# Delta rule and two FFNs on one core: when the second FFN's weights are prepared

## What is computed

```python
# 1: delta rule, B 4, H 8, S 768, D 48
k_n = k / (norm(k) + 1e-6)
for t in range(S):
    y[:, :, t] = einsum('bhd,bhde->bhe', q[:, :, t], state)
    v_old = einsum('bhde,bhd->bhe', state, k_n[:, :, t])
    state = state + beta[t] * einsum('bhd,bhe->bhde', k_n[:, :, t], v[:, :, t] - v_old)
x = y as (3072 tokens, 384)
# 2: first FFN, d_ff 2048
h = maximum(x @ w_in, 0.0);  x = (h * h) @ w_out
# 3: second FFN, d_ff 1536
out = (1 / (1 + exp(-(x @ w_gate))) * (x @ w_val)) @ w_last
```

## Time and profile before

| | us |
|---|---|
| median of 3 runs (lowest, highest) | 992.91 (991.66, 994.58) |
| the profiled execution's own time | 993.12 |
| its span | 991.3 |
| PE busy | 946.8 (96%) |
| DVE busy | 655.4 (66%) |
| ACT busy | 515.1 (52%) |
| POOL busy | 12.4 (1%) |
| mean granted clock of PE, of full speed | 0.987 |

### The profile page before, as it was taken

One profiled execution on the slowest core, in us unless ns is written; L12 is line 12 of the kernel. 1 busy time (PEld: TensorE's weight loads), 2 busy tenths in 40 slices (PEclk: granted clock), 3 DMA queues, 4 the chain that ended last, 5 costly groups with the idle time before them and its releaser, 6 DMA issues.

```text
span 991.3 us, 24647 instructions
## 1 busy us (share of the span) xinstructions
PE 946.8 (96%) x10372; PEld 518.8 (52%) x10372; DVE 655.4 (66%) x1260; ACT 515.1 (52%) x903; POOL 12.4 (1%) x27
## 2 busy tenths in 40 slices
PE   2878999999999999999999999999999999999998
PEld 1464555565565456556544445555555555555554
DVE  7998966965866885694236744675565655756745
ACT  4896655766576476556669843233333333232332
POOL 0000000000000000000000000000000000000000
PEclk7899999999999999999999999999999999999999
DMA  9633016024003202201133010010010010100000
GB/s 311 127 81 84 2 35 129 34 67 96 34 19 81 67 33 66 65 33 41 59 121 135 1 64 1 1 63 0 0 63 0 0 63 0 35 28 0 32 1 33
DMA packets 21001, 52.23 MB, mean 53 GB/s; under 512 B 2672, under 2 KB 12912, under 8 KB 20528
## 3 DMA queue, kind: packets, MB, share of 16 engines
q1 hardware_dynamic: 20320, 50.60, 18.0%
q10 hardware_dynamic: 592, 0.33, 0.1%
HBM read 41.48 MB, written 9.44 MB: 51 GB/s over the span
## 4 chain that ended last, share of the span: by engine, by line
PE 83%; DVE 9%; ACT 3%; issue 3%; DMA 1%; SPq 0%; POOL 0%; DVEq 0%; POOLq 0%; ACTq 0%
PE psum L699 72%; PE psum L613 2%; DMA raw_a<-in_w_in 1%; ACT work L833 1%; PE psum L600 1%; DVE attn L1212 1%; PE psum L570 1%; DVE attn L1210 1%; PE psum L557 1%; PE psum L582 1%; PE psum L628 1%; PE psum L544 1%; PE psum L642 1%; PE psum L509 1%; DVE work L1256 1%
## 5 line engine op out<-in xcount | busy, mean ns | idle before, releaser
L699 PE MATMUL psum<-work,w 128*128 128x512 f16 x1728 | 387.9, 381 | 9.6 <-DVE work L1256 4.1
L699 PE MATMUL psum<-attn 128*128 128x512 f16 x1296 | 285.4, 379 | 0.0
L699 PEld LDWEIGHTS psum<-work,w 128*128 128x128 f16 x1728 | 164.7, 98 | 206.3 <-issue 8.2
L833 ACT ACTIVATE work<-work 128x512 f16<-128x512 f32 (+1 forms) x264 | 155.8, 624 | 154.4 <-DVE work L1459 150.8
L699 PEld LDWEIGHTS psum<-attn 128*128 128x128 f16 x1296 | 126.8, 98 | 145.7 <-DVE attn L1285 1.3
L1459 DVE SCALAR_TENSOR_TENSOR work<-psum,work 128x512 f32<-128x512 f32 x72 | 49.8, 691 | 134.5 <-PE psum L699 120.2
L833 ACT ACTIVATE work<-psum,scal 128x512 f32<-128x512 f32 x90 | 60.1, 682 | 81.4 <-PE psum L699 81.4
L1256 DVE SCALAR_TENSOR_TENSOR work<-work 128x512 f16<-128x512 f16 x96 | 65.7, 689 | 52.1 <-ACT work L833 50.7
L833 ACT ACTIVATE attn<-psum 64x384 f32<-64x384 f32 (+5 forms) x160 | 65.8, 441 | 50.6 <-PE psum L570 21.0
L833 ACT ACTIVATE work<-psum 128x512 f32<-128x512 f32 x96 | 57.0, 594 | 66.7 <-PE psum L699 65.6
L699 PE MATMUL psum<-work,attn 128*128 128x256 f16 (+1 forms) x540 | 87.9, 315 | 0.0
(11 more groups left out here) (119 smaller groups left out, 747.3 us busy)
## 6 DMA issues: line engine op xcount, KB each, us to landing
attn<-in_kt SPq DMA_DIRECT2D x24, 192.0 KB, 4.0
attn<-in_v SPq DMA_DIRECT2D x24, 192.0 KB, 3.9
attn<-in_kn SPq DMA_DIRECT2D x24, 192.0 KB, 3.9
x_spill<-work SPq DMA_DIRECT2D x6, 768.0 KB, 3.3
xt<-x_spill SPq DMA_DIRECT2D x6, 768.0 KB, 5.0
attn<-in_qt SPq DMA_DIRECT2D x20, 192.0 KB, 4.3
y_out<-work SPq DMA_DIRECT2D x5, 768.0 KB, 3.6
work<-in_w_out SPq DMA_DIRECT2D x1, 3072.0 KB, 24.1
```

What stands on the lines that cost most here:

```text
L699: m = mm(dst, x, z, start=first and i == 0, stop=last and i == len(a) - 1)
L833: return nc.scalar.activation(out, in_, f, scale=scale)
```

## The change

In stage 5 (`GROUPS - 1`), ACT now calls `second_weights(k - 18)` and DVE `second_weights(k - 19)` at the odd steps up to 35, so that the arguments -4 to -1 (ACT) and -3 and -2 (DVE) fall there; in stage 6 DVE starts at argument -1. The calls are put at other arguments: w_gate four earlier (its cuts one to each argument), w_val two earlier, w_last one earlier, and the split of x2 goes from argument 12 to 13. No other engine's code is touched.

```diff
--- before.py
+++ after.py
@@ -976,27 +976,26 @@
                 run(hi[:, at], raw[:, at], scale=cell(at_cell + 2)).then_inc(w_hi_done, 1)
 
             def second_weights(k):
-                if k == 0:
+                if k == -4:
                     weight_squares(raw_a[:, 0:part2], WG, attn[:, 0:part2], "wg", 16)
+                if k == -3:
+                    weight_root(2, WG)
+                if -2 <= k < PIECES - 2:
+                    cut_second(2, k + 2, raw_a[:, 0:part2], WG, w2p[0])
                 if k == 1:
-                    weight_root(2, WG)
-                if k in (2, 3):
-                    for n in ((0, 1), (2,))[k - 2]:
-                        cut_second(2, n, raw_a[:, 0:part2], WG, w2p[0])
-                if k == 3:
                     weight_squares(raw_b, WV, attn[:, part2:2 * part2], "wv", 16)
-                if k == 4:
+                if k == 2:
                     weight_root(3, WV)
-                if 5 <= k < 5 + PIECES:
-                    cut_second(3, k - 5, raw_b, WV, w2p[2])
+                if 3 <= k < 3 + PIECES:
+                    cut_second(3, k - 3, raw_b, WV, w2p[2])
+                if k == 7:
+                    weight_squares(raw_a[:, 0:part2], WL, attn[:, 2 * part2:3 * part2], "wl", 16)
                 if k == 8:
-                    weight_squares(raw_a[:, 0:part2], WL, attn[:, 2 * part2:3 * part2], "wl", 16)
-                if k == 9:
                     weight_root(4, WL)
-                if 10 <= k < 10 + PIECES:
-                    cut_second(4, k - 10, raw_a[:, 0:part2], WL, w2p[4])
-                if k in (11, 13):
-                    combined_high(k == 13)
+                if 9 <= k < 9 + PIECES:
+                    cut_second(4, k - 9, raw_a[:, 0:part2], WL, w2p[4])
+                if k in (10, 12):
+                    combined_high(k == 12)
 
             def combined_high(n):
 
@@ -1042,7 +1041,9 @@
                             cut_small(n)
                     if s < GROUPS - 1 and step == place(s, "norm" if s else "root"):
                         root_k(s + 1)
-                    if s == GROUPS and second:
+                    if s == GROUPS - 1 and second and 0 <= step < STEPS:
+                        second_weights(k - N1 - LAG)
+                    if s == GROUPS and second and k >= 0:
                         second_weights(k)
 
             act.dma_start(beta_s[:], beta.rearrange("p g u -> p (g u)")).then_inc(in_beta, 16)
@@ -1318,27 +1319,26 @@
                     .then_inc(w_out_done, 1)
 
             def second_weights(k):
-                if k == 1:
+                if k == -3:
                     weight_scale(2, WG)
-                if k in (2, 3):
-                    for n in ((0, 1), (2,))[k - 2]:
-                        cut_rest_second(2, n, raw_a[:, 0:part2], WG, w2p[0], w2p[1])
-                if k == 4:
+                if -2 <= k < PIECES - 2:
+                    cut_rest_second(2, k + 2, raw_a[:, 0:part2], WG, w2p[0], w2p[1])
+                if k == 2:
                     weight_scale(3, WV)
-                if 5 <= k < 5 + PIECES:
-                    cut_rest_second(3, k - 5, raw_b, WV, w2p[2], w2p[3])
-                if k == 9:
+                if 3 <= k < 3 + PIECES:
+                    cut_rest_second(3, k - 3, raw_b, WV, w2p[2], w2p[3])
+                if k == 8:
                     weight_scale(4, WL)
                     combine_first()
-                if 10 <= k < 10 + PIECES:
-                    cut_rest_second(4, k - 10, raw_a[:, 0:part2], WL, w2p[4], w2p[5])
+                if 9 <= k < 9 + PIECES:
+                    cut_rest_second(4, k - 9, raw_a[:, 0:part2], WL, w2p[4], w2p[5])
+                if k == 9:
+                    scale_x2(0)
+                if k in (10, 12):
+                    combined_rest(k == 12)
                 if k == 10:
-                    scale_x2(0)
-                if k in (11, 13):
-                    combined_rest(k == 13)
-                if k == 11:
                     combine_second()
-                if k == 12:
+                if k == 13:
                     split_x(x2_split, GROUPS, x2_hi, x2_lo)
 
             def quarters():
@@ -1427,7 +1427,9 @@
                         if step == place(s, "start"):
                             coefficients(s + 1)
                             start_lanes(s + 1)
-                    if s == GROUPS and odd and k >= 1:
+                    if s == GROUPS - 1 and odd and 0 <= step < STEPS:
+                        second_weights(k - 1 - N1 - LAG)
+                    if s == GROUPS and odd and k >= 0:
                         second_weights(k - 1)
 
             dve.sem_inc(glo_ready, 2)
```

## The result

The changed kernel takes 996.62 us (median of 19 runs, 994.59 to 998.87), the kernel before on the same chips 994.75 us (19 runs, 991.44 to 995.70). The ratio is 1.0027, 95% interval 1.0019 to 1.0034: slower by 2.7 us, the size and the sign that were forecast. The interval reaches to both sides of the 0.3% that was called the bound of "slower"; the ratio itself lies just under it. The ratio is not the quotient of the two medians, which lie 1.9 us apart (0.19%); the two means lie 2.8 us apart (0.28%). One of the 12 executions of experiment 4 took 5568 us and is left out of its ratio.

What follows compares the result with a forecast made beforehand. PE, busy 946.8 of 991.3 us, was taken as the bound. New stops of 6.65 us less old 5.6 us gave +1.1 us; the clock's +1.6 us made +2.7 us on 992.9: 995.6 us, range 993.4 to 997.9.

Steps and rivals of the forecast that it cites:

- new stop at `hidden(2)`: Stage 6, PE: waits for the Relu of k = 0, delayed by the later read-out of x2; 0.45 us.
- new stop at `hidden(4)`: Stage 6, PE: waits for the Relu of k = 2 while ACT stands behind w_val's load; 6.1 us.
- the five old stops: Stage 6, PE: two stops released by ACT and three by DVE, all but about 0.1 us to go; 5.6 us.
- Step 1: Stage 5, ACT: w_gate's squares behind k = 14 cost nothing, with 0.4 us of cover left before DVE's L1256.
- Step 2: ACT: w_gate's scale and two cuts delay the x2 read-out by 1.7 us; new 0.45 us PE stop, old 0.55 us stop goes.
- Step 3: Stage 6: w_val's squares moved behind k = 1; ACT waits 5.0 us for its load, PE stops 6.1 us, 1.68 us stop goes.
- Step 4: End of stage 6: with the remaining work spread evenly, three DVE stops shrink from 2.55 us to about 0.1 us.
- Step 5: PE's clock: falls to half once at the 6.1 us stop, costing +1.6 us, bounds 0 and 3.3 us.
- The rival of a shared queue: w_last's load shares the queue with w_val's, lengthening PE's stop by 4.6 us: +7.3 us, 1000.2; chance 0.05.
- The rival of a clock that holds: PE's clock stays full through the long stop: +1.1 us, 994.0; chance 0.15.
- The rival of a clock that stays down longer: PE's clock stays down twice as long behind the long stop: +4.4 us, 997.3; chance 0.15.
- The faster rival: Stage 6: w_val's data land within 4.2 us of issue, in time for ACT: -4.0 us, 988.9; chance 0.03.

Runs made afterwards that it cites:

- experiment 4: Kernel before with only w_last's work one argument earlier and the split of x2 one later: ratio 0.9992 against the kernel before.
- experiment 1: Changed kernel with SP issuing w_val's load ahead of the x2 store that waits for the read-out: ratio 0.9963 against the kernel before.
- experiment 3: Changed kernel with w_val's squares, root and cuts put back two arguments later, as in the kernel before: ratio 0.9966 against the kernel before.
- experiment 10: Changed kernel with SP also waiting for the x2 store to land before issuing w_val's load: ratio 1.0053 against the kernel before.
- experiment 7: Kernel before with only w_val's load issued ahead of the store of x2: ratio 1.0004 against the kernel before.
- experiment 5: Kernel before with only w_gate's part of the change; w_val, w_last and the split of x2 as before: ratio 0.9969.
- experiment 2: Changed kernel with 27 dummy matmuls on PE ahead of the wait of `hidden(4)` in stage 6: ratio 1.0010 against the kernel before.
- experiment 9: Changed kernel with 13 dummy matmuls on PE ahead of `hidden(4)`, run twice: ratios 1.0034 and 1.0037 against the kernel before.
- experiment 6: Changed kernel with w_val's squares, root and cuts one argument later: ratio 0.9982 against the kernel before.
- experiment 8: Changed kernel with w_val's load issued ahead of the x2 store and w_val's work one argument later: 988.79 us, ratio 0.9951.

## Why the prediction was right, step by step

The forecast was +2.7 us and 995.6 us; the ratio says +0.27% and the stretch +2.70 us. By its own terms, each stop with the 0.16 us for filling and draining:

| term | predicted us | measured us |
|---|---|---|
| new stop at `hidden(2)` | 0.45 | 0.17 + 0.16 = 0.33 |
| new stop at `hidden(4)` | 6.1 | 5.89 + 0.16 = 6.05 |
| stops near the end | 0.1 | none |
| the five old stops | -5.6 | -5.6, all five gone |
| lower clock | +1.6 | +1.79 |
| sum | +2.7 | +2.6 |

The steps are right, but that the sum hits so closely is in part luck. The stretch less the clock's 1.79 us leaves 0.9 us for the stops, where 1.1 us were forecast, and the clock was forecast 0.2 us too low: the two misses cancel. The median of 996.62 us lies 1.0 us above the 995.6, because I started from the median of three executions, 992.91, which is 994.75 over nineteen. The table's measured sum is 0.1 us under the stretch; these rows do not resolve that rest.

- *Step 1, squares of w_gate in stage 5.* Right. The Relu of k = 15 went at 503.43, with its squares done at 505.19, and DVE came to L1257 at 505.6: 0.4 us of cover, and the first stop kept its 0.89 us.
- *Step 2, cuts ahead of the read-out.* Right: 1.66 us later against 1.7. The stop at `hidden(2)` had 0.17 us of idle time, under the 0.3 to 0.5 us that I named as its sign.
- *Step 3, the wait for w_val.* Right, and it carries the result. Experiments 1, 3 and 10 move the load or the squares alone and the stop follows; experiment 7 shows that the load's time is free where ACT is later than the data.
- *Step 4, the even spread.* The three DVE stops vanished, 0.1 us was expected to stay. But experiment 4 shows that this is not the spread's own work: alone it gains 0.19 us. It works only together with the moves of w_gate and w_val: w_gate's move without it (experiment 5) leaves two of the three stops, and w_gate's move and the spread with w_val where it was (experiment 3) leave one of 1.40 us. That the two moves help by letting ACT come early to w_last's squares is my reading.
- *Step 5, the clock.* Right in kind, and experiment 2 isolates it. It was mis-sized by 0.2 us: I took one low stretch of nine matmuls from the earlier trace rows, 3.4 us; here 3.6 us of work fell under the low clock and 1.79 us were lost. By my own sign, a low clock of over 3.4 us, this step is just missed, and the low clock as a whole lasted 6.8 us, nearly half of it inside the stop.
- *The rival of a shared queue* falls: w_val landed 9.0 us after issue with w_last 4.3 us behind it, against 9.2 us before, where w_last was issued only after it had landed. In experiment 10 it landed in 8.2 us with w_last issued 1.6 us behind, as fast as in experiment 1, where the next issue came 18.7 us later. The Trainium skill, DMA: Bandwidth & Descriptors, section Queues, rings and completion order, says that each engine takes the descriptors of a ring in order; the rows agree, and the load behind took longer instead: 11.0 us here and 12.9 in experiment 10.
- *The rival of a clock that holds* was too simple: experiment 9 shows both outcomes for one program, behind a stop half as long. For the stop of 5.9 us only one profile exists, with the clock fallen.
- *The rival of a clock that stays down longer* did not come in the profile of the change, but the longer stop of experiment 10 went part of the way: 2.47 us lost, where the rival had 3.3.
- *The faster rival* needed a landing within 4.2 us; the fastest of w_val in any run was 8.1 us (experiment 7).

Where 4.8 us of idle time could be had, the change had nearly all of it in hand and gave it back at one wait, since it moved the consumer of a DMA without moving its issue.

## What to carry to other kernels

When work moves forward in one engine's program, list every producer it waits for and look where each of those is issued in its own queue: here the slack was 5.4 us, and ACT wanted w_val 8.9 us earlier while its data came 1.4 us later (both counted from the first row of PE's timeline). A long stop of PE can be paid for twice, once in the stop and again in the half clock behind it (6.1 and 1.8 us here; experiment 9 kept its clock once), so one long stop can cost more than several short ones of the same sum. And a spread that gains nothing by itself (experiment 4) may still be needed by another part: try the parts alone and together.

## What the runs showed of the hardware that was not expected

- A stop of 2.07 us was followed by the half clock in one profile, which fell about 0.9 us after PE had gone on (experiment 6), while stops of 1.83 us were not, and stops of 3.22 and 3.26 us went both ways in two executions of one program. The length of the stop alone does not decide it.
- The low clock is also part of the scatter between executions: with the same instructions ahead of it, stage 5 ended between 506.28 and 509.41 us in the profiles shown, and at 126 us one profile ran at half clock where another ran at full.
- With a store of 768 KB issued 0.6 us ahead of it, the 2304 KB load of w_val landed 9.0 to 9.2 us after its issue in all nine profiles that have this order; without one (experiments 1, 7, 8 and 10) it landed after 8.1 to 8.4 us. A load 1.6 us behind it showed no cost (8.2 us, experiment 10). The load of w_last took 11.0 to 11.2 us in the seven profiles where it was issued 4.3 us behind that of w_val; with w_val long landed it took 8.8 to 9.1 us in four profiles, but 10.6 in experiment 4, for which I have no reason.
- SP's issue of the load of x2 took 2.67 us with two loads of 2304 KB still under way, and 4.53 us in experiment 10, where both had been issued within 2.1 us; before, with one under way, it took 0.79 us.
